# Routing inside the delta rule, late zeroing of tails, and transposes of h behind the second layer

## The reference

```python
for t in range(S):
    kt, vt, bt = (k_n[:, :, t], v[:, :, t], beta[:, :, t, None])
    y[:, :, t] = np.einsum('bhd,bhde->bhe', q[:, :, t], state)
    v_old = np.einsum('bhde,bhd->bhe', state, kt)
    state = state + bt[:, :, :, None] * np.einsum('bhd,bhe->bhde', kt, vt - v_old)
```

## Time and profile before

| | us |
|---|---|
| median of 3 runs | 1154.94 (1149.84 to 1159.45) |
| the profiled execution | 1154.56 |
| its span, first to last instruction | 1152.8 |
| TensorE busy | 1012.1, 88% |
| VectorE / ScalarE / GpSimd busy | 482.1 / 366.7 / 324.4 |

### The profile page before, as it was taken

How to read it: one execution, slowest core, us unless ns; L and a number is a source line. 1 busy time by engine, 2 the same in 40 slices (tenths; PEclk the granted TensorE clock), 3 DMA queues, 4 the chain that set the end, 5 groups by cost and what they waited for, 6 DMA issues and landing times. The chain is left out here.

```text
span 1152.8 us, 30762 instructions
## 1 busy us (share of the span) xinstructions
PE 1012.1 (88%) x13236; PEld 887.3 (77%) x13236; DVE 482.1 (42%) x922; ACT 366.7 (32%) x731; POOL 324.4 (28%) x226
## 2 busy tenths in 40 slices
PE   1789999999998999810899999999599999999999
PEld 1678878888887888710799999999578888888888
DVE  3455555555555554360344344344242314242321
ACT  0255545555554555410222222222121212122211
POOL 2232333233422421046545255453420101000000
PEclk9999999999999999955899999999889999999999
DMA  8712121220212100016324344432211000100000
GB/s 267 269 54 63 28 60 40 62 63 26 63 40 62 41 20 19 2 42 232 136 81 155 122 151 151 150 124 82 89 49 35 28 34 20 34 20 28 10 19 28
DMA packets 59394, 86.37 MB, mean 75 GB/s; under 512 B 29200, under 2 KB 54288, under 8 KB 56720
## 3 DMA queue, kind: packets, MB, share of 16 engines
q1 hardware_dynamic: 53616, 48.46, 13.1%
q0 software_dynamic: 5664, 36.18, 9.2%
HBM read 61.82 MB, written 22.81 MB: 73 GB/s over the span
## 5 line engine op out<-in xcount | busy, mean ns | idle before, releaser
L1029 PE MATMUL hb<-early,last_h 128*128 128x512 f32 x648 | 203.8, 396 | 4.7 <-ACT o_sb L1143 3.5
L1029 PEld LDWEIGHTS hb<-early,last_h 128*128 128x128 f32 x648 | 120.5, 189 | 30.8 <-ACT o_sb L1143 2.7
L1029 PE MATMUL hb<-early,last_l 128*128 128x512 f32 x324 | 126.9, 392 | 0.0
L480 DVE TENSOR_TENSOR p<-bank,cf 128x512 f16<-128x512 f32 x96 | 66.0, 688 | 45.1 <-PE bank L283 44.8
L283 PEld LDWEIGHTS bank<-t,n_hi 64*64 64x64 f16 x2688 | 66.2, 111 | 21.1 <-issue 5.7
L1167 DVE TENSOR_TENSOR m<-hb,m 128x512 f32<-128x512 f32 x36 | 24.9, 691 | 131.4 <-PE hb L1029 131.4
L283 PE MATMUL bank<-t,n_hi 64*64 64x64 f16 x2688 | 71.6, 195 | 4.6 <-issue 3.9
L1029 PE MATMUL ob<-wo_h,early 128*128 128x384 f32 x288 | 74.2, 335 | 0.0
L1029 PEld LDWEIGHTS hb<-early,last_l 128*128 128x128 f32 x324 | 61.3, 189 | 13.2
L951 POOL TENSOR_TENSOR late<-w_raw,late 128x3072 fp32r<-128x3072 f32 x8 | 54.4, 6801 | 56.3 <-DVE late L923 56.0
L585 POOL COPY x_all<-y_tile 128x384 f32<-128x384 f32 x24 | 12.1, 503 | 205.3 <-ACT y_tile L451 205.3
(11 more groups left out here) (155 smaller groups left out, 2191.4 us busy)
## 6 DMA issues: line engine op xcount, KB each, us to landing
w_raw<-w POOLq DMA_DIRECT2D x14, 1536.0 KB, 7.6
kq_t<-qh SPq DMA_DIRECT2D x24, 256.0 KB, 3.3
x_sorted<-zeros SPq DMA_DIRECT2D x32, 192.0 KB, 1.9
x_in<-x_sorted SPq DMA_DIRECT2D x29, 192.0 KB, 2.4
y_sorted<-y_sb SPq DMA_DIRECT2D x28, 192.0 KB, 1.9
k_raw<-kt_in SPq DMA_DIRECT2D x24, 192.0 KB, 3.5
k_own<-kh SPq DMA_DIRECT2D x24, 192.0 KB, 3.3
v_in<-vh SPq DMA_DIRECT2D x24, 192.0 KB, 3.3
```

What stands on the lines that cost most here:

```text
L480: dve.tensor_tensor(p16[st][:], pb, mask_of(lv), ALU.mult).then_inc(prod_out[st], 1)
L1029: ins = pe.matmul(out, a[x], b[y], start=first and i == 0, stop=last and i == 2, skip_group_check=True)
```

## The change

- `route_and_sort` is gone. In the delta rule CHAIN gets three pieces behind the logits: in lg VectorE also finds the chosen expert of the tile (best, score, top, chosen); rank is two small float16 matmuls, a triangular matrix times this tile's choice and an all-ones matrix times the running count; slot makes the row numbers and adds to the count; send is GpSimd's indirect DMA of the tile, straight from `y_tile`, which gets two buffers. `x_all` and its copy are gone.
- Row numbers can be known at once because each expert has an area of 26 tiles of its own in `x_sorted`. The first chain product of the next step waits for slot's first operation (`routed`) instead of the logits copy. In `walk` the pieces of older steps come first within a slot.
- Nothing is zeroed up front. When the counts are known, SyncE zeroes two tiles behind expert 0's last token, and in the experts' stage those of expert e + 1 while expert e runs. Each expert gets at least 2 tiles. 14 spare tiles of `y_sorted` are zeroed, spread over the steps.
- The logits product has 16 columns instead of 128.
- Expert 0's weights are split in six pieces in steps 2 to 7 (NORM parts 10, 11, 12), and expert 1's are loaded in step 10 (part 13).
- After the delta rule there is one totals product and ten VectorE operations for the table. The gate values are computed at the start of the experts' stage.
- In the experts the transposes of h follow the whole second layer of the tile in front, and the cast of the second half of h no longer waits for `y_done`. Blocks of `y_sorted` stand LEAD = 3 tiles behind the loop, and the row numbers are moved by as much.

```diff
 F2 = 768
-MAXB = TILES + E - 1
+MINB = 2
+MAXB = TILES + (E - 1) * MINB
 EPS = 1e-6
 
...
-    CHAIN = {0: ("ks", 0), 2: ("z", 0), 4: ("up", 0), 6: ("ks", 1), 8: ("z", 1), 10: ("up", 1), 12: ("yt", 0), 14: ("lg", 0)}
-    NORM = {1: [0], 2: [1], 3: [2], 5: [3], 6: [4], 7: [5], 8: [6], 9: [7, 8], 10: [9]}
+    CHAIN = {0: ("ks", 0), 2: ("z", 0), 4: ("up", 0), 6: ("ks", 1), 8: ("z", 1), 10: ("up", 1), 12: ("yt", 0), 14: ("lg", 0),
+             15: ("rank", 0), 16: ("slot", 0), 17: ("send", 0)}
+    NORM = {1: [0], 2: [1], 3: [2], 4: [10], 5: [3], 6: [4], 7: [5], 8: [6], 9: [7, 8], 10: [9], 12: [11], 13: [13], 14: [12]}
...
-                for of, off in ((a, 0), (c, SLOTS), (b, 2 * SLOTS)):
+                for of, off in ((b, 2 * SLOTS), (c, SLOTS), (a, 0)):
...
         sp.wait_ge(zeros_ready, 1)
-        with sp.Fori(0, MAXB + 1) as g:
-            sp.dma_start(xs[bass.ds(P * g, P), :], zeros[:]).then_inc(xs_zeroed, 16)
-
-        with sp.Fori(TILES, MAXB + 1) as g:
-            sp.dma_start(ys[bass.ds(P * g, P), :], zeros[:]).then_inc(xs_zeroed, 16)
-
         for raw, arrived, w in zip(weights.raw, weights.raw_in, (w1, w2)):
             sp.dma_start(raw[:], w[0]).then_inc(arrived, 16)
         load_k(2, 0)
@@ -273,6 +300,15 @@
             if k + 1 < STEPS:
                 load_k(k + 1, (k + 1) % 2)
             load_qv(k, k % 2)
+            for i in range(BLANK * (k - 2) // (STEPS - 2), BLANK * (k - 1) // (STEPS - 2)):
+                at = P * (LEAD + TILES + i)
+                sp.dma_start(ys[at:at + P, :], zeros[:]).then_inc(zeroed, 16)
+        sp.wait_ge(zeroed, 16 * BLANK)
+        sp.wait_ge(tabled, 8)
+        row = sp.value_load(table[0:1, 2, 0:1], min_val=0, max_val=N)
+        sp.dma_start(xs[bass.ds(row, MINB * P), :].rearrange("(n p) x -> p n x", p=P),
+                     zeros[:].unsqueeze(1).broadcast_to((P, MINB, X))).then_inc(zeroed, 16)
+        sp.wait_ge(zeroed, 16 * BLANK + 16)
...
-                    pe.wait_ge(logit_out[st], k)
+                    pe.wait_ge(routed[st], 5 * k - 1)
...
-                    ins = pe.matmul(out[:, X:X + P], y_t[st][:, c, :], wr[:, c, :], start=c == 0, stop=c == KX - 1,
+                    ins = pe.matmul(out[:, X:X + 2 * E], y_t[st][:, c, :], wr[:, c, :], start=c == 0, stop=c == KX - 1,
...
+            elif what == "rank":
+                pe.wait_ge(chosen_ready[st], k + 1)
+                if 2 * k + st >= 1:
+                    pe.wait_ge(counted_ready, 2 * k + st)
+                pe.sem_inc(passed_pe, 1)
+                pe.matmul(out[:, X + P - E:X + P], tri16, chosen[:, 2 * k + st, :], start=True, stop=False, skip_group_check=True)
+                pe.matmul(out[:, X + P - E:X + P], ones16, counted[:], start=False, stop=True,
+                          skip_group_check=True).then_inc(rank_done[st], 1)
...
+        pe.wait_ge(counted_ready, TILES)
+        pe.sem_inc(passed_pe, 1)
+        pe.matmul(bank[0][0][:, 0:E], ones16, counted[:], start=True, stop=True, skip_group_check=True).then_inc(totals_done, 1)
...
-                if e == 0 and k >= 1:
-                    act.wait_ge(x_out[st], k)
-                act.copy(y_tile[st][half[e], :], yb[st][C:P, 0:X]).then_inc(y_out[st], 1)
+                if e == 0 and k >= 2:
+                    act.wait_ge(rows_sent[st], 16 * (k - 1))
+                act.copy(y_tile[par][st][half[e], :], yb[st][C:P, 0:X]).then_inc(y_out[st], 1)
...
             elif what == "lg":
                 dve.wait_ge(logit_done[st], k + 1)
-                dve.tensor_copy(logits[:, 2 * k + st, :], yb[st][:, X:X + 2 * E]).then_inc(logit_out[st], 1)
+                to = 2 * k + st
+                dve.tensor_copy(logits[:, to, :], yb[st][:, X:X + 2 * E]).then_inc(logit_out[st], 1)
+                dve.wait_ge(logit_out[st], k + 1)
+                dve.tensor_reduce(best[:, st:st + 1], logits[:, to, 0:E], AX.X, ALU.max).then_inc(routed[st], 1)
+                dve.wait_ge(routed[st], 5 * k + 1)
+                dve.scalar_tensor_tensor(out=score[st][:], in0=logits[:, to, 0:E], scalar=best[:, st:st + 1],
+                                         in1=cf[:, CF_IOTA:CF_IOTA + E], op0=ALU.is_equal, op1=ALU.mult).then_inc(routed[st], 1)
+                dve.wait_ge(routed[st], 5 * k + 2)
+                dve.tensor_reduce(top[:, st:st + 1], score[st][:], AX.X, ALU.max).then_inc(routed[st], 1)
+                dve.wait_ge(routed[st], 5 * k + 3)
+                dve.tensor_scalar(chosen[:, to, :], score[st][:], top[:, st:st + 1], None, ALU.is_equal).then_inc(chosen_ready[st], 1)
+            elif what == "slot":
+                to = 2 * k + st
+                dve.wait_ge(rank_done[st], k + 1)
+                dve.tensor_tensor(place[st][:], yb[st][:, X + P - E:X + P], chosen[:, to, :], ALU.mult).then_inc(routed[st], 1)
+                dve.wait_ge(routed[st], 5 * k + 4)
+                dve.tensor_reduce(slot_f[:, to:to + 1], place[st][:], AX.X, ALU.add).then_inc(routed[st], 1)
+                dve.wait_ge(routed[st], 5 * k + 5)
+                dve.tensor_copy(rows_at[:, to:to + 1], slot_f[:, to:to + 1]).then_inc(slot_ready[st], 1)
+                dve.tensor_tensor(counted[:], counted[:], chosen[:, to, :], ALU.add).then_inc(counted_ready, 1)
...
+            elif part in (10, 11, 12) and 2 <= k < 2 + PIECES:
+                if k == 2 and part == 10:
+                    for i in range(2):
+                        dve.wait_ge(weights.raw_in[i], 16)
+                cols = slice((k - 2) * KX * F // PIECES, (k - 1) * KX * F // PIECES)
+                i = part - 11
+                if part == 10:
+                    for raw, (hi, lo), ready in zip((0, 1), first_split, weights.hi_ready):
+                        ins = dve.tensor_copy(hi[:, cols], weights.flat_raw(raw)[:, cols])
+                        if k == 1 + PIECES:
+                            ins.then_inc(ready, 1)
+                        else:
+                            ins.then_inc(piece_done, 1)
+                else:
+                    if k == 1 + PIECES:
+                        dve.wait_ge(weights.hi_ready[i], 1)
+                    else:
+                        dve.wait_ge(piece_done, 2 * (k - 2) + 1 + i)
+                    hi, lo = first_split[i]
+                    ins = dve.tensor_tensor(lo[:, cols], weights.flat_raw(i)[:, cols], hi[:, cols], ALU.subtract)
+                    if k == 1 + PIECES:
+                        ins.then_inc(weights.lo_ready[i], 1)
...
+        dve.wait_ge(totals_done, 1)
+        dve.tensor_tensor(more[:], bank[0][0][:, 0:E].unsqueeze(2).broadcast_to((P, E, TILES)),
+                          cf[:, CF_STEP:CF_STEP + E * TILES].rearrange("p (e t) -> p e t", e=E), ALU.is_gt).then_inc(tabled, 1)
+        dve.wait_ge(tabled, 1)
+        dve.tensor_copy(table[:, 2], bank[0][0][:, 0:E])
+        dve.tensor_reduce(blocks[:], more[:], AX.X, ALU.add).then_inc(tabled, 1)
+        dve.wait_ge(tabled, 2)
+        dve.tensor_scalar(blocks[:], blocks[:], float(MINB), None, ALU.max).then_inc(tabled, 1)
+        dve.wait_ge(tabled, 3)
+        dve.tensor_tensor(sums[:], blocks[:].unsqueeze(1).broadcast_to((P, E, E)),
+                          cf[:, CF_SUM:CF_SUM + E * E].rearrange("p (a b) -> p a b", a=E), ALU.mult).then_inc(tabled, 1)
+        dve.wait_ge(tabled, 4)
+        dve.tensor_reduce(ends[:], sums[:], AX.X, ALU.add).then_inc(tabled, 1)
+        dve.wait_ge(tabled, 5)
+        dve.tensor_copy(table[:, 1], ends[:])
+        dve.tensor_tensor(begins[:], ends[:], blocks[:], ALU.subtract).then_inc(tabled, 1)
+        dve.wait_ge(tabled, 6)
+        dve.tensor_tensor(shift[:], cf[:, CF_AREA:CF_AREA + E], begins[:], ALU.subtract).then_inc(tabled, 1)
+        dve.wait_ge(tabled, 7)
+        dve.tensor_copy(table[:, 0], shift[:]).then_inc(tabled, 1)
...
-            if what == "yt":
-                pool.wait_ge(y_out[st], 2 * k + 2)
-                pool.tensor_copy(x_all[:, 2 * k + st, :], y_tile[st][:]).then_inc(x_out[st], 1)
+            if what == "send":
+                to = 2 * k + st
+                pool.wait_ge(slot_ready[st], k + 1)
+                if k >= 1:
+                    pool.wait_ge(rows_sent[st], 16 * k)
+                pool.indirect_dma_start(xs, bass.IndirectOffsetOnAxis(ap=rows_at[:, to:to + 1], axis=0),
+                                        y_tile[par][st][:], None).then_inc(rows_sent[st], 16)
...
+            elif part == 13 and k == STEPS - 2:
+                for i, w in enumerate((w1, w2)):
+                    pool.wait_ge(weights.lo_ready[i], 1)
+                    pool.dma_start(weights.raw[i][:], w[1]).then_inc(weights.raw_again[i], 16)
...
-
-
-def route_and_sort(nc, ctx, sems, cf, x_all, logits, gate, slots, table, xs, xs_zeroed, weights, w1, w2):
...
+        for st in range(2):
+            pool.wait_ge(rows_sent[st], 16 * STEPS)
+
+
+def experts(nc, ctx, sems, cf, routing, gate, slots, xs, ys, weights, w1, w2, w_in, w_out):
...
+        def tile(e, g, off):
+            sp.wait_ge(xt_done, g)
```

(62 more changed lines are left out.)

246 lines of the change are left out of this document (79 added, 167 removed).

## The result

The changed kernel took 1209.74 us (median of 4 runs, 1203.37 to 1214.72); the kernel before took 1157.20 us on the same chip. The ratio is 1.0455, 95% interval 1.0373 to 1.0537: slower by 4.5%, where 1121.4 us and faster were forecast.

The account below looks back on a forecast made before the run. It took GpSimd's scatter queue to bound the hole and TensorE the other stages. Hole -44.2, TensorE +4, VectorE +8, SyncE -1, experts 0 sum to -33.2: 1154.6 becomes 1121.4 us, own range 1113 to 1134.

Parts of the forecast that it names:

- The hole: Between the last logits copy and the experts' first product: scatters move into the delta rule, 44.2 us go.
- The step that failed: GpSimd in the delta rule: loses a copy, gains a scatter of 0.97 to 2.96 us per tile; cost to TensorE nothing.
- TensorE +4: Delta rule: two rank matmuls per tile less the narrower logits products, net 0.15 x 24, +4 us (-2 to +7).
- VectorE +8: Delta rule: small operations and split pieces delay TensorE 0.2 us for each of 24 tiles and 18 pieces; bounds 0 to 52.
- The stage's forecast of +11: Delta rule as a whole: TensorE +4, VectorE +8, SyncE's dropped zero writes -1 us.
- the prediction's walk: Delta rule's 16 slots walked through: logits choice and rank product delay masks, so TensorE loses 0.1 to 0.2 us.
- The last layer "untouched": Last layer after the experts: untouched by the change, 0 us.
- Experts 0: Experts' stage: moved transposes and casts leave tiles 9.51 us apart, 0 us (-1 to +2).
- D: Delta rule: GpSimd and VectorE block each other in SBUF, 81 us in place of the 8, 1194 us; chance 0.04.
- B: Delta rule: VectorE late in many slots, +25 to +42 us instead of 8, 1138 to 1155 us; chance 0.09.
- C: Hole shrinks only to 20 to 25 us, last scatter or zero tail being slow: 1128 to 1133 us; chance 0.07.

Follow-up runs that it names:

- experiment 1: Changed kernel with GpSimd's send of stream 0 at slot 18 of CHAIN instead of 17 (stream 1's also one later): 1146.36 us, ratio 0.9876 to the kernel before.
- experiment 3: Kernel before with GpSimd's copy of the result tile moved to slot 17, waiting for the next step's first chain product, older steps first: 1229.88 us, ratio 1.0595.
- experiments 7 and 8: 7: kernel before, two unused tiles giving nearly the changed layout, 1168.0 us; 8: changed kernel, send at 18, padded to the earlier layout, 1132.34 us.

## Why the prediction was wrong

- **The hole: right.** -44.9 us for -44.2, and each intermediate step within 1 us.
- **The step that failed** is the sentence on GpSimd: "the sends stand in slots 2 and 11, ahead of work needed slots later: nothing". It priced the send's issue (about 1 us, right) and not its wait. The send waits for VectorE's row numbers of the slot just in front, GpSimd waits with it (254.9 us in 23 waits; before it was 205.3 in 24, but not in this place), and what is queued behind is `kb`. That work is indeed needed late by its own reader; but SyncE's queue waits for it with q and v of the present step behind. Followed one engine further, the prediction would have found it: of the 6.5 us between the issue of q and its use the loads of q and v take about 4, and the 2.4 left were all the slack there was, against waits of GpSimd of 7 us and more. Price: 53.0 us of waits at one line, and with the lower clock 73.4 us of this stage, by experiment 1 (the ratios of the whole runs make it some 67); 71.0 by experiment 3.
- **The clock was left out of the delta rule.** The forecast let TensorE wait at full clock. Of +96.9 us 38.3 are the same work at a lower granted clock (0.90 for 0.99). A stop of 5.8 us was followed by products of nearly twice the time, and so was one of 1.4 us in a thin stretch.
- **TensorE +4 and VectorE +8:** with the send out of the way the stage is +23.5 us, some 10 idle and 13 busy, in a profile whose clock reads 0.97. The work itself was sized well (busy time by clock equal within some 4 us; VectorE +44.6 us for 52), and masks don't stop TensorE longer than before (5.6 us for 8.4). The stage's forecast of +11 reads +15 to +32 in the profiles of the variants whose sends don't hold up the loads, and these profiles differ in their clocks. With the send at 18, 3.5 us of it are the rank product's waits for the choice, 0.15 per tile, as the prediction's walk had them. How much of the rest belongs to the pieces and how much to the routing stays open.
- **The last layer "untouched":** its instructions are, its addresses are not. +7.6 us, by experiments 7 and 8.
- **Experts 0:** +0.6, and the moved transposes alone 1.0001. Right. That the tiles are no longer 9.51 us apart is the place in SBUF again, and not the new order: 9.50 with the order alone, and 9.50 with both and the layout of before.
- **The rivals.** D gave the right sign at 1194 us and by the wrong mechanism: the new small operations of VectorE took what they should. The logits' choice, 24 times, in after:

```profile
L558 DVE TENSOR_SCALAR chosen<-score,top x24: 231/231/232, 92.5 to 591.6; 128x8 f16<-128x8 f32 x24
```

The two engines met seldom, as forecast (beta_k: median 161 ns of 48, longest 1,840, as before). By the Trainium skill, GPSIMD Engine Reference, "Key points", GpSimd and VectorE contend in their SBUF interfaces when VectorE has two SBUF inputs. The trace agrees where they do meet: one piece of the split took 1.81 us beside GpSimd's squares of the keys, the like one 0.68 us a little later.

```profile
135.34 1.81 DVE L627 TENSOR_TENSOR early<-w_raw,early 128x512 fp32r<-128x512 f32 x1
...
139.63 0.68 DVE L627 TENSOR_TENSOR early<-w_raw,early 128x512 fp32r<-128x512 f32 x1
```

But contention was the wrong thing to fear between the two: the queue was. B (late masks) and C (a slow scatter or zero tail) didn't happen. The chance of 0.04 for slower was far too small: a wait moved to a new place of an in-order queue was in the change, and no rival was made from it.

## What to carry to other kernels

When a change puts a waiting instruction into an engine's queue, write down what stands behind it, who waits for that, and what stands behind those waits on the next engine, until the chain ends at the bounding engine; compare its slack with the length of the wait. Here moving the instruction one slot, behind the urgent work, turned a loss of 4.5% into a gain of 1.2%, and 2.5% with the layout. Price a stop of TensorE at more than its length: the products after it may run at half clock (they did after the 1.4 us at 199.4 with the send at 18, and not after the 1.9 us at 370.9 in the kernel before). And after any change of allocations compare the mean time of untouched products: if all are longer by the same share, look at where the tiles lie before looking for a wait.

## What was unexpected of the hardware

- The same 648 products of 128x512 took 396 ns in the mean with their weights' tiles at one place in SBUF and 402 or 403 at another, at the same granted clock (0.99), in the same program; over the last layer 312.3 to 313.9 us against 319.0 to 321.0, and per expert tile 9.50 us against 9.49 to 9.61 with the layout of after. Moving the kernel before by pads alone brought it on, padding the changed one took it away. A pad of 32 bytes alone was worth about 1 us at most.
- TensorE stopped for 1.2 to 5.1 us inside runs of like products, where the program has no wait. All 52 such stops of over 1.2 us ended 1.3 to 1.6 us after a 16 KB packet landed on the queue called instruction. The stops of 3.4 us and more all fell beside a 3 MB load, in four of the seven kernels that have it there.
- Granted clock and time go together from run to run of one kernel: 1127.7 us at 0.972, 1141.3 at 0.962.
